# Delta rule with its small products in 32-row tiles, y turned by identity products, and the last rounds of the inverses on VectorE

## What is computed

```python
# q, k, v: (4, 8, 768, 48), beta: (4, 8, 768)
k_n = k / (np.linalg.norm(k, axis=-1, keepdims=True) + 1e-06)
state = np.zeros((B, H, D, D))
for t in range(S):
    y[:, :, t] = einsum('bhd,bhde->bhe', q[:, :, t], state)
    v_old = einsum('bhde,bhd->bhe', state, k_n[:, :, t])
    state = state + beta[:, :, t] * einsum('bhd,bhe->bhde', k_n[:, :, t], v[:, :, t] - v_old)
x = y as (B * S, H * D)
x = (P(h) / Q(h)) @ w_out      # h = x @ w_in, 3072 x 384 x 2048
out = mish(x @ w2_in) @ w2_out
```

## Time and profile before

| | us |
|---|---|
| median of 3 runs | 1170.5 (1156.2 to 1177.8) |
| the profiled execution | 1173.3 |
| its span | 1171.5 |
| TensorE busy in the span | 1071.8 (91%) |
| VectorE busy | 950.9 (81%) |
| ScalarE busy | 766.7 (65%) |
| GpSimd busy | 171.6 (15%) |

### The profile page before, as it was taken

The page is one execution under the profiler, slowest core; times in us unless marked ns, Lnnn a source line. Parts: engine busy times, 40 slices in busy tenths (PEclk is TensorE's granted clock), DMA queues, the critical chain, the costliest instruction groups (busy, mean ns, idle before and its releaser), DMA issues.

```text
span 1171.5 us, 22278 instructions
## 1 busy us (share of the span) xinstructions
PE 1071.8 (91%) x9321; PEld 870.6 (74%) x9366; DVE 950.9 (81%) x1045; ACT 766.7 (65%) x1039; POOL 171.6 (15%) x328
## 2 busy tenths in 40 slices
PE   5388999999888899999999999889999999999997
PEld 3276877877766677787787777668888888888885
DVE  4965567554569999999999999999887888878785
ACT  1535456466367687777867768687676767667664
POOL 2088787780000000000000000000000000000000
PEclk7588889996899999999999999999999999999999
DMA  7625447343021010000101003230010101010000
GB/s 198 185 62 159 137 111 192 97 110 124 22 87 54 1 55 1 25 30 0 54 0 54 1 1 108 81 107 28 1 55 1 54 0 54 1 54 1 25 4 27
DMA packets 30489, 69.03 MB, mean 59 GB/s; under 512 B 4160, under 2 KB 11840, under 8 KB 30400
## 3 DMA queue, kind: packets, MB, share of 16 engines
q1 hardware_dynamic: 30144, 66.98, 19.2%
q10 hardware_dynamic: 256, 0.79, 0.3%
HBM read 53.60 MB, written 14.16 MB: 58 GB/s over the span
## 4 chain that ended last, share of the span: by engine, by line
DVE 35%; PE 33%; issue 3%; ACT 2%; DVEq 0%; ACTq 0%
PE o_ps L837 6%; PE o_ps L838 5%; PE o_ps L839 5%; PE h_ps L837 5%; PE h_ps L839 5%; PE h_ps L838 5%; DVE val L1022 5%; DVE val L1041 5%; DVE val L1054 5%; DVE g_lo L1060 5%; DVE den L1014 5%; DVE den L1049 5%; DVE pa L1020 4%; PE h_ps L881 0%; ACT den L901 0%
## 5 line engine op out<-in xcount | busy, mean ns | idle before, releaser
L910 ACT ACTIVATE g_hi<-val 128x1024 fp32r<-128x1024 f32 x96 | 102.0, 1062 | 99.7 <-DVE val L1054 93.6
L837 PE MATMUL o_ps<-g_hi,w_hi_late 128*128 128x512 f32 x288 | 116.8, 405 | 20.5 <-DVE g_lo L1060 20.4
L837 PE MATMUL o_ps<-g_hi,w_hi_early 128*128 128x512 f32 x288 | 114.8, 399 | 14.3 <-ACT stage L947 9.2
L1054 DVE SCALAR_TENSOR_TENSOR val<-den,val 128x1024 f32<-128x1024 f32 x96 | 117.7, 1226 | 10.7 <-DVE den L1049 0.5
L1060 DVE SCALAR_TENSOR_TENSOR g_lo<-val,g_hi 128x1024 fp32r<-128x1024 f32 x96 | 117.6, 1225 | 1.6 <-ACT g_hi L910 1.5
L837 PE MATMUL h_ps<-x_hi,w_hi_early 128*128 128x512 f32 x288 | 112.2, 390 | 2.0 <-DVE val L1022 2.0
L837 PE MATMUL h_ps<-x_hi,w_hi_late 128*128 128x512 f32 x288 | 112.5, 391 | 1.6 <-DVE w_lo_late L88 1.6
L838 PE MATMUL o_ps<-g_lo,w_hi_late 128*128 128x512 f32 x288 | 113.8, 395 | 0.0
L839 PE MATMUL o_ps<-g_hi,w_lo_early 128*128 128x512 f32 x288 | 113.5, 394 | 0.0
L838 PE MATMUL o_ps<-g_lo,w_hi_early 128*128 128x512 f32 x288 | 113.4, 394 | 0.0
L839 PE MATMUL o_ps<-g_hi,w_lo_late 128*128 128x512 f32 x288 | 113.3, 393 | 0.0
(11 more groups left out here) (111 smaller groups left out, 2360.2 us busy)
## 6 DMA issues: line engine op xcount, KB each, us to landing
w_raw<-w SPq DMA_DIRECT2D x16, 768.0 KB, 6.1
kv_run<-kv_n SPq DMA_DIRECT2D x24, 384.0 KB, 4.6
x_raw<-x_dram SPq DMA_DIRECT2D x12, 768.0 KB, 5.8
kq_run<-kq_t SPq DMA_DIRECT2D x44, 192.0 KB, 3.5
kq_gram<-kq_t SPq DMA_DIRECT2D x40, 192.0 KB, 6.7
x_dram<-stage SPq DMA_DIRECT2D x24, 192.0 KB, 4.0
x_dram<-stage SPq DMA_DIRECT2D x6, 768.0 KB, 4.3
out<-stage SPq DMA_DIRECT2D x5, 768.0 KB, 4.1
```

Of the source, the lines that this page charges most:

```text
L837: nc.tensor.matmul(dst, hi, rhs_hi, start=first, stop=False)
L910: act_fn(g_hi[:, n % 2], val[:, n % 2], ACT.Copy, scale=-1.0).then_inc(g_hi_ready, 1)
L1054: dve_stt(val[:, e], den[:, e], 2.0, val[:, e], ALU.subtract, ALU.mult).then_inc(g_ready, 1)
```

## The change

`solve`, `q_state`, `k_state` and `within` are now all 16 products, each for one head and one batch, with 32 columns of weights and 48 columns moving. `solve` and `within` use the four diagonal tiles of 32x32 (rows and columns of `quad(b)`), with `x_mat` and `p_mat` themselves as weights; so `x_blk`, `p_blk`, `u_row` and ScalarE's spreading go. `q_state` has q as weights and the state moving, as `k_state` has k. `update` stays as it was.

y comes out with positions in the partitions, in the upper half of the two banks that also hold `ks` (`ky_ps`). There is one place for it: `q_state` waits for the copy of the y of the step before, and `within` also waits for the next step's z, since VectorE reads the same banks. ScalarE copies y into `y_tok`, TensorE turns it one step later by two products with the identity as the moving operand (`turn_y`), and ScalarE copies that into `y_stage` (`copy_turned`), which is stored with one transfer for each half tile.

k and q are loaded once, into a ring of three tiles that serves the gram and the steps. The warming products have a bank of their own, stand only ahead of `update`, and are one instead of two.

The inverses of tiles 1 to 5 are shared: GpSimd makes rounds 31 to 9, VectorE rounds 8 to 1, placed by hand in steps 5 to 7 ahead of (`FRONT`) and behind (`BACK`) `add_state`; for tile 1 all eight stand behind step 7. `turn_x` moves behind step 7, `root_inverse` to step 4, and `weights(1)` behind the inverse of tile 0.

```diff
+Y_AT = BANK // 2
-WARM = 2
+WARM = 1
+TAIL = 8
+FRONT = [(), (), (), (), (), (8,), (5,), (2, 1)]
+BACK = [(), (), (), (), (), (7, 6), (4, 3), ()]
...
-        def substitute(eng, tt, j, own, step, done):
+        def rounds(eng, tt, j, own, step, done, first, last):
-            for r in range(C - 1, 0, -1):
+            for r in range(first, last, -1):
...
+            sp.wait_ge(ident_zeroed, 1)
+            for b in range(B):
+                sp.dma_start(ident[quad(b), quad(b)],
+                             consts[0:1, C + B:C + B + C * C].rearrange("o (i k) -> (o i) k", k=C)).then_inc(ident_loaded, 16)
+            sp.wait_ge(gram_done, 4)
             for c in range(CT):
-                load_gram(1, c)
+                for r in range(HALVES):
+                    load_kq(sp, 1, c, r)
...
-                substitute(pool, nc.gpsimd.tensor_tensor, j, 0, inv_step, STEPS * (j - 1))
+                rounds(pool, nc.gpsimd.tensor_tensor, j, 0, pool_step, (STEPS - TAIL_STEPS) * (j - 1), C - 1, TAIL)
...
             def solve(tau, c, g):
                 for u in range(U):
-                    last = nc.tensor.matmul(hz_ps[:, u], x_blk[:, c, U * g + u], z[:, g, u],
-                                            start=True, stop=True)
+                    for b in range(B):
+                        last = nc.tensor.matmul(hz_ps[quad(b), D * u:D * u + D],
+                                                x_mat[quad(b), tau % 2, HEADS * c + U * g + u],
+                                                z[quad(b), g, u], start=True, stop=True)
...
             def q_state(tau, c, g):
-                for s in range(V * B):
-                    for r in range(HALVES):
-                        nc.tensor.matmul(y_ps[g][half(r), s // B, s % B], state[rows(r), g, D * s:D * s + WIDE],
-                                         kq_run[rows(r), c, 1, B * V * g + s],
-                                         start=(s == 0), stop=False, skip_group_check=True)
+                if q:
+                    pe.wait_ge(y_copied, q)
+                    by_event()
+                for v in range(V):
+                    for b in range(B):
+                        for r in range(HALVES):
+                            last = nc.tensor.matmul(y_at(r, v, b), kq[rows(r), slot(tau, c), 1, B * (V * g + v) + b],
+                                                    state[rows(r), g, v, b],
+                                                    start=(v == 0), stop=False, skip_group_check=True)
...
             def within(tau, c, g):
-                pe.wait_ge(u_ready, q + 1)
+                pe.wait_ge(q_done, q + 1)
+                if q + 1 < NQ * T:
+                    pe.wait_ge(z_ready, q + 2)
+                for v in range(V):
+                    for r in range(HALVES):
+                        for b in range(B):
+                            last = nc.tensor.matmul(y_at(r, v, b), p_mat[quad(b), tau % RING, HEADS * c + U * g + V * r + v],
+                                                    u_blk[quad(b), g, V * r + v, b],
+                                                    start=False, stop=True, skip_group_check=True)
...
+            def turn_y(q):
+                pe.wait_ge(y_copied, q + 1)
+                for r in range(HALVES):
+                    last = nc.tensor.matmul(turn_ps[0:V * D, P * r:P * r + P], y_tok[:, q % 2, r], ident[:],
+                                            start=True, stop=True)
...
                     solve(tau, c, g)
-                    if gram:
+                    if tau + 2 < T and 0 <= fill < 4:
                         gram_fill(tau + 2, fill)
                     q_state(tau, c, g)
...
+                    if q:
+                        turn_y(q - 1)
+                    keep_warm(warm_ps[:], WARM)
                     update(tau, c, g)
                     within(tau, c, g)
...
+            def last_rounds(j, some):
+                for r in some:
+                    if r == TAIL:
+                        dve.wait_ge(inv_ready, j)
+                    rounds(dve, dve_tt, j, 1, dve_step, STEPS + TAIL_STEPS * (j - 1) + 2 * (TAIL - r), r, r - 1)
...
+                    if tau and tau + 1 < T:
+                        last_rounds(tau + 1, FRONT[s])
                     add_state(tau, c, g)
...
+                    if tau and tau + 1 < T:
+                        last_rounds(tau + 1, BACK[s])
+                    if (tau, s) == (0, NQ - 1):
+                        last_rounds(1, range(TAIL, 0, -1))
-                    if fill == 6 and tau + 1 < T:
+                    if s == NQ - 1 and tau + 1 < T:
                         turn_x(tau + 1, 0, half_k)
```

More of the change, by code:

```diff
@@ L334, in _, with keep_warm @@
             busy = idle[:].bitcast(mybir.dt.bfloat16)
+            def keep_warm(bank, n):
+                for _ in range(n):
+                    nc.tensor.matmul(bank, busy[:, 0:P], busy, start=True, stop=True)
             def gram_fill(j, f):
                 cp, r = f // 2, f % 2
-                if j == 0 and r == 0:
+                if r == 0:
                     for c2 in range(2):
-                        pe.wait_ge(kq_loaded[2 * cp + c2], 32)
-                if j and r == 0:
-                    for c2 in range(2):
-                        pe.wait_ge(kq_gram_loaded[2 * cp + c2], 32 * j)
+                        pe.wait_ge(kq_loaded[slot(j, 2 * cp + c2)], 32 * (j // RING) + 32)
+                if (j, f) == (1, 3):
+                    pe.wait_ge(gram_used, 4)
                 if j >= 2:
@@ L352, in gram_fill @@
                         for b in range(B):
-                            kq = operands[rows(r), 2 * cp + c2, :, B * s + b, :]
-                            last = nc.tensor.matmul(fill[quad(b), :, c2, s // V, s % V], kq[:, 0], kq,
+                            both = kq[rows(r), slot(j, 2 * cp + c2), :, B * s + b, :]
+                            last = nc.tensor.matmul(fill[quad(b), :, c2, s // V, s % V], both[:, 0], both,
                                                     start=True, stop=True)
                 last.then_inc(gram_done, 1)
-            def keep_warm(n):
-                for _ in range(n):
-                    nc.tensor.matmul(gram_bank[:], busy[:, 0:P], busy, start=True, stop=True)
             def k_state(tau, c, g):
@@ L401, in update @@
                 keys = kv_run[:, c].rearrange("p a h d -> p (a h d)")
-                for u, r, v in slots:
-                    h = U * g + u
-                    last = nc.tensor.matmul(st_ps[g][half(r), v].rearrange("p b d -> p (b d)"),
-                                            keys[:, D * h:D * h + WIDE],
-                                            u_blk[:, g, u].rearrange("p b d -> p (b d)"), start=True, stop=True)
+                for v in range(V):
+                    for r in range(HALVES):
+                        u = V * r + v
+                        at = D * (U * g + u)
+                        last = nc.tensor.matmul(st_ps[g][64 * r:64 * r + WIDE, v].rearrange("p b d -> p (b d)"),
+                                                keys[:, at:at + WIDE],
+                                                u_blk[:, g, u].rearrange("p b d -> p (b d)"), start=True, stop=True)
                 last.then_inc(st_done, 1)
@@ L455, in _ @@
                         k_state(tau + 1, 0, 0)
-                    if not gram:
-                        if tau + 2 < T and fill == 4:
-                            pe.wait_ge(gram_used, 4 * (tau + 2) + 4)
-                        keep_warm(WARM)
+                    if q:
+                        turn_y(q - 1)
+                    keep_warm(warm_ps[:], WARM)
                     update(tau, c, g)
                     within(tau, c, g)
+            turn_y(NQ * T - 1)
         @block.scalar
@@ L693, in _ @@
             root_inverse(1)
-            weights(1)
             scale_gram(0, 3)
@@ L704, in _ @@
             spread_w(0)
+            weights(1)
             for f in range(4):
```

337 lines of the change are left out of this document (147 added, 190 removed).

## The result

The changed kernel takes 1211.2 us as the median of four runs (1206.8 to 1215.2), the kernel before 1174.2 in the same comparison (1156.2 to 1181.9). The ratio is 1.041, with a 95% interval from 1.028 to 1.054. Here and in all that follows the medians take in every execution, but the ratios leave out those over 1.5% above the fastest of their kernel, so that 1.041 is more than 1211.2 / 1174.2 = 1.032. The forecast of 1132 and its range to 1180 were wrong, and so was their sign.

A forecast was written before the change was run, and what follows sets the result against it. TensorE was taken to bound plain steps of the delta rule, VectorE only where extra work falls. Terms -44 - 9 - 4 - 2 + 21 = -38 us gave 1132 us against the median 1170.5, range 1105 to 1180.

The forecast's parts named there:

- Sum of a step: ... = 3.27, so 0.91 less; 48 steps: -44: TensorE's parts of an undisturbed full-clock step, summed to 3.27 us instead of 4.18: -44 us over 48 steps.
- If the low clock covers the same ten steps ... -9: TensorE's steps at the low clock: 5.7 us instead of 7.52, another 0.9 for each of ten: -9 us.
- VectorE's operations on SBUF can be late beside a running GpSimd ... some 0.05 each: 4 (bounds 0, 12): VectorE's inverse rounds: 80 operations, each some 0.05 us late beside GpSimd, costing 4 us, bounds 0 and 12.
- 5.0 + 2.4: First tile boundary: eight inverse rounds and the turn of x in the open, 7.4 us against 5.6 before: 1.8 lost.
- 4.6 + 4 + 1.8: Sharing on VectorE: rounds sticking out over four tiles 4.6 us, lateness beside GpSimd 4, first boundary 1.8.
- The row of `w_blk` at 0.77: VectorE, profile row cited for lateness beside GpSimd: `w_blk`, smaller than a `z` of 0.35, took 0.77 us.
- fourteen half transposes and half sums at 0.3: VectorE: half transposes of N and half sums, 14 of them, stick out by 0.3 us, given as 4.5.
- The third rival: Low clock spreads in the loop: 1166 us with 24 low steps, 1204 with 40; sign mean clock under 0.8; chance 0.20.
- the first rival: VectorE or GpSimd becomes the bound, their waits on each other in order: 1152 us; chance 0.16.
- lateness: First rival's surviving case: only lateness of VectorE and GpSimd adds, four tiles five us longer: 1152 us.
- The diagonal tiles of one bank: Second rival, solve and within: diagonal tiles run one behind the other, 1.5 us each, 1228 us; chance 0.08.

The follow-up runs named there:

- a_fewer: Changed kernel with solve and within moving the same columns in a quarter of the products, output not the reference's: 1167.3 us, ratio 0.997 to the kernel before.
- a_pool: Changed kernel with all rounds of the inverses back on GpSimd, none on VectorE: 1200.4 us, ratio 1.024 to the kernel before.
- a_fewer_pool: Changed kernel with a quarter of the products in solve and within and all inverse rounds on GpSimd, output wrong: 1146.7 us, 0.976 of the kernel before.
- a_lean: Changed kernel with most k, q and v loads cut to a sixteenth, output not the reference's: 1199.2 us, ratio 1.022 to the kernel before.

## Why the prediction was wrong

**What failed first: "Sum of a step: ... = 3.27, so 0.91 less; 48 steps: -44" had no term for the fetching of TensorE's instructions.** The loop, from the first to the last `u_blk`, grew from 259.2 to 303.8 us. The sum counted columns and weights for each form, and most came out: within and the wait for y, which hides solve, 1.08 (1.03 predicted), solve 0.52 (0.5), the turn with the warming product 0.82 (0.77), update 0.80 (0.87); only q_state and k_state together are longer, 0.90 (0.6; 0.73 in a_fewer). An undisturbed step is 3.6 us, 3.42 in a_fewer, against 3.27. But the change makes 16 small products of four in solve and within, and these 256 instructions in 2.1 us are what the fetching doesn't follow: 61.3 us of stalls where the kernel before has 2.6. The low clock that follows adds its part, and the term "If the low clock covers the same ten steps ... -9" failed with it; a_fewer measures both together as 44 to 52. The rows of before could have raised the question: q_state and k_state there issue 128 in 1.5 us without a stall, next to groups of 1 us with 8 records, and nothing in the step was then as dense for 2 us.

**What failed second: "VectorE's operations on SBUF can be late beside a running GpSimd ... some 0.05 each: 4 (bounds 0, 12)".** The 64 operations of rounds that ran beside GpSimd took 12.9 us more than the same 16 shapes in tile 4, where GpSimd had ended: 0.20 each and beyond the bound of 12. At the first boundary 14 of 16 take 0.59 to 0.67, from 192 elements down to 31, where alone they are 0.36 to 0.19; in the next three tiles the sixteen take 2.2 to 3.0 us more. The first boundary, with 7.4 in the open ("5.0 + 2.4") predicted at 10.7 with its step of 3.27, took 98.66 to 119.90, 21.2 between two `u_blk`, of which 2.9 are a stall in q_state and 10.5 the rounds (106.39 to 116.93) that alone took 5.0; with all rounds on GpSimd this interval is 7.3 (a_pool). In all the sharing costs 11 to 20 us in the stalled kernel and 16 to 25 in the other, where the prediction had 10.4 for it (4.6 + 4 + 1.8). The row of `w_blk` at 0.77, which stood in the prediction, was the sign: alone the same operation takes 0.28 in the kernel after, so it was lengthened by 0.5 and not by 0.05. A slip beside it changes little: fourteen half transposes and half sums at 0.3 are 4.2 and not 4.5.

**The low clock.** The third rival's sign came true, 0.79 in the loop's stage and 133 instead of 72 us, and so did its direction. Its reason mostly did not: it put the cause on the warming product, smaller tiles and idle tile ends, but two more warming products change no time, and a_fewer is at 68 us with one, on the same tiles.

**The other rivals.** VectorE is no bound in plain steps, and its list of waits has no row that names GpSimd, so the first rival's ring of waits isn't there; its "lateness" is, in the second point above. The diagonal tiles of one bank run side by side: 32 records in 0.52 us, not 1.5, and in a_fewer 8 records of 192 columns in 0.50, where update's 8 of 192 columns on the whole array take 0.87. The Trainium skill's sentence on row tiles and one bank (TensorEngine Tiling (Array Packing), Restrictions and Gotchas) does not hold for tiles that write different partitions of it.

**What would the sum have been?** a_fewer_pool has the new step without most stalls and without the sharing. It is 28 us faster than the kernel before, where the forecast without the sharing's 10.4 would be 48 faster. The missing 20 are as much as the stalls that it has more (22.2 against 2.6); that they are the same 20 was not shown. From there the sharing gives back 21 and the instructions 44: -28 + 21 + 44 = +37, the loss by the medians (1211.2 less 1174.2). This has to come out, as the terms are differences along one row of kernels, and is no proof of its own; by the ratios it is -28 + 25 + 52 = +49. Between the groups of runs the kernel before alone differs by up to 8 us, so the terms are good to about that.

**What stays open.** How many instructions lie fetched ahead, and so where the limit is between the kernel before and the one after, no run shows. An estimate says why so little is left over: the undisturbed step issues 284 records in 3.61 us, a packet of some 250 in 3.2 us, and in the loops of all fourteen traces no two packets start less than 3.2 us apart. Where the 20 us that a_fewer_pool lacks against the forecast lie is open too.

## What to carry to other kernels

Where a change splits products, count its instructions as well as its columns: a group that issues a few hundred in two microseconds needs its own term, and the sign of a shortage is idle time under "issue" in the middle of a group together with more packets in the instruction queue. Short operations of VectorE that showed this delay should be priced from rows that were measured beside a busy GpSimd: each can wait for the rest of GpSimd's running operation, here up to 0.5 us. In this kernel the low clock behind the stalls went when the stalls did; warming products cost about what they gave back.

## What the hardware showed unexpectedly

- Four diagonal 32x32 tiles with 48 columns are as fast in 32 records (0.52 us) as in 8 records of 192 columns (0.50): in an undisturbed step the small products cost nothing.
- TensorE's program comes in packets of 16 KB while it runs, some 250 instructions each, and a stall ends 1.2 to 1.8 us behind the landing of one. Data transfers delay them: the stall of 4.7 us lies under a burst of 96% busy engines, and cutting the traffic (a_lean) took 13 us off the stalls without making them fewer.
- VectorE's products and subtractions of two operands in SBUF wait for GpSimd's running operation: up to 0.67 us for 31 to 192 elements, against 0.19 to 0.36 alone. The same does not happen to `z`, `add_state` and `u_blk`, which read a bank (0.35, 0.55 and 0.96 beside GpSimd and alone), nor to RECIPROCAL (0.35) and the transposes (1.1 each).
- With small products in place of the two warming ones (b_many) the mean granted clock of the kernel before falls from 0.86 to 0.78, though TensorE is busy 92% of the stretch, more than the 90% of the earlier trace rows; its 14 us of stalls are not told apart from this. Its windows row:

```profile
59.80:361.20 301.40, 278.50 (x7324) 239.07 (x7312) 152.15 (x288) 136.24 (x406) 165.34 (x318) 0.78 0.37 99
```
